# Attention scores from raw fp32 queries and keys in quarter-array tiles, values as the stationary operand, rows divided before the transposes

## The chip, the cores and the metric

The kernel runs on one core of a Trainium2 chip. The metric is the device time of the whole program in microseconds (us). The engines are PE (TensorE: matmul; PEld: its weight loads), DVE (VectorE), ACT (ScalarE), POOL (GpSimd) and SP, which here only issues transfers. Two executions of this kernel count as different from about 0.3%.

## The reference, cut to what matters

```
q, k, v: (4 batches, 8 heads, 576 positions, 64) fp32
scores = q k^T / 8
kth    = 32nd largest of each row of scores
scores = where(scores >= kth, scores, -1e9) - row maximum
attn   = exp(scores);  attn = attn / (sum(attn) + 1e-9)
x      = (attn v), heads side by side: 2304 rows x 512
h = x w_in (512x2048);  g = h / (1 + exp(-1.702 h));  x2 = g w_out (2048x512)
out = (((x2 w1) * (x2 w2)) w3) w_out2      (w1, w2: 512x1024; w3: 1024x1024; w_out2: 1024x512)
```

Row `kth` needs the scores close to full fp32 precision, since a wrong choice among near-equal scores changes the result.

## The kernel before, in words

The 2304 rows are eight chunks of 288 queries. A chunk is 18 tiles of 128 score rows: two groups of four heads, each with one "left" tile (the last 32 queries of all four heads) and eight full tiles (one head, 128 queries). One tile has 128 rows of 576 scores. The loops of all engines go by slots, one per tile; in a slot each engine does its share for several tiles at different stages: PE makes the scores of the tile two ahead, DVE searches the current and the previous one, ACT and POOL mask and exponentiate the tile two behind, and PE transposes the probabilities and weighs the values of the tile three behind. Each slot also holds one or two of the 32 units of the first feed-forward block, for the chunk before (12 fp16 matmuls a unit); units 0 to 15 give hidden rows and need a tanh, a gate product on DVE (L1014) and a split in high and low parts (ACT L865, POOL L1250); units 16 to 31 multiply by w_out. The first chunks carry other work in their place: the product of the two last weights on PE, peaks and splits of the weights on DVE. The order is written out by hand in each engine's `step`; engines meet only by counting semaphores. The search on DVE is four MAX8 and three MATCH_REPLACE8 over the 576 scores of a tile. After all chunks the second feed-forward block runs in six blocks of 384 rows, a stage of its own.

Scores (L545 to 564). Queries and keys arrive with the 64 head dimensions on partitions, twice, on both halves (L372). ACT rounds them to fp32r with a mask over the halves (`round_q`, `round_k`, L738 to 755), and POOL subtracts to get the low parts (`prepare`, L1198), so that one stationary holds high and low parts on 128 rows, and the stacked keys hold both too. A full tile is then two stationaries by two halves of the keys: four matmuls of 288 columns. A left tile needs sixteen. These preparations run nine tiles ahead, in slots 0 to 5 of each nine.

Values (L577 to 591). The transposed probabilities (L566; five transposes in a tile, copied from PSUM by ACT in two pieces, L798 and L799) are the stationary operand, the values the moving one: five fp32 matmuls of 64 columns in a full tile, 256 in a left tile. Each fp32 matmul stands as two in the records. ACT scales the result by the inverse sum (`copy_output`, L802 to 819), PE transposes it into x_T (`transpose_x`, L593), ACT takes the high part (L821) and DVE the low part (L1023). In the first chunk SP waits for the splits before it loads the next queries into the single buffer (L380).

Of the kernel before, what the change touches and what calls it, by code (L numbers as in the profile page):

```python
# [19 lines left out]
FP32 = mybir.dt.float32  # L20
# [3 lines left out]
ALU = mybir.AluOpType  # L24
# [14 lines left out]
NT = CT * NCHUNK  # L39
KB = S // P  # L40
# [78 lines left out]
class Tile:  # L119


    def __init__(self, chunk, s):
        self.chunk, self.s = chunk.next(s // CT), s % CT
        self.fixed = CT * self.chunk.off + self.s
        self.g, self.r = self.s // GT, self.s % GT
        self.left = self.r == 0
        self.h, self.j = self.g * HG + (self.r - 1) // 2, (self.r - 1) % 2
# [13 lines left out]
    def makes_xt(self):  # L141

        return self.left or self.h % 2 == 1

    def xt_count(self, extra=0):

        before = sum(Tile(Chunk(0), i).makes_xt() for i in range(self.s))
        return self.chunk.count(XT, before + extra)


XT = sum(Tile(Chunk(0), i).makes_xt() for i in range(CT))
# [52 lines left out]
def build(nc, q_in, k_in, v_in, w_in_d, w_out_d, w1_d, w2_d, w3t_d, wo2_d, out_d, x2_d, w3o_d):  # L204
# [14 lines left out]
    kst = sb("k_stack", [P, 2, HG, S], FP32R)  # L219
    kx = sb("k_stage", [P, HG, S], FP32)  # L220
    vn = sb("v_rows", [P, KB + 1, DM], FP32)
    qx = sb("q_stage", [P, HG, CHUNK], FP32)
    qs = [sb("q_high_low", [P, 2, HG, FULL], FP32R), sb("q_low_high", [P, 2, HG, FULL], FP32R)]

    DIAG = P + LEFT
    ql = [sb("q_left_high_low", [P, 2, HG * DIAG], FP32R), sb("q_left_low_high", [P, 2, HG * DIAG], FP32R)]
    attn_end = place[0]
# [5 lines left out]
    pt = sb("probs_T", [P, (KB + 1) * P], FP32)  # L233
    xn = sb("x_rows", [P, 2, 2, P], FP32)
    xl = sb("x_left", [P, 2, P], FP32)
# [17 lines left out]
    low_rows = sb("low_rows", [P, 2], FP32)  # L253
# [17 lines left out]
    at = pinned["k_stack"]  # L271
# [23 lines left out]
    ptp = nc.alloc_psum_tensor("probs_T_ps", [P, 512], FP32)  # L295
    pte = nc.alloc_psum_tensor("probs_T_end_ps", [P, 512], FP32)
    xp = nc.alloc_psum_tensor("values_ps", [P, 512], FP32)
    xtp = nc.alloc_psum_tensor("x_T_ps", [P, 512], FP32)
    mp = [nc.alloc_psum_tensor(f"ff_ps{i}", [P, 512], FP32) for i in range(2)]
    yp = [ps[:, 0, :], ps[:, 1, :], xp[:, :]]  # L300

    sem = nc.alloc_semaphore
    q_loaded, k_loaded, v_loaded = sem("q_loaded"), sem("k_loaded"), [sem("v_loaded0"), sem("v_loaded1")]
# [6 lines left out]
    q_rounded, k_rounded = sem("q_rounded"), sem("k_rounded")  # L310
    q_split, k_split = sem("q_split"), sem("k_split")
    edge_set = sem("edge_set")
    ident_set, zeros_set, rows_set = sem("ident_set"), sem("zeros_set"), sem("rows_set")
# [4 lines left out]
    transposed, pt_copied, av_done, o_copied = sem("transposed"), sem("pt_copied"), sem("av_done"), sem("o_copied")  # L318
    xt_made, xt_high, xt_low = sem("xt_made"), sem("xt_high"), sem("xt_low")
# [12 lines left out]
    def new_keys(tile):  # L332

        return tile.chunk.off % 2 == 0

    def xt_parts(t, dst):

        par = t.chunk.off % 2
        if not t.left:
            return [(slice(0, P), dst[:, par, t.h // 2, t.j * P:(t.j + 1) * P], xtp[:, 0:P])]  # L340
        parts = []
        for odd in range(2):
            rows = slice(odd * D, (odd + 1) * D)
            parts.append((rows, dst[rows, par, 2 * t.g:2 * t.g + 2, FULL:CHUNK],
                          xtp[rows, 0:P].rearrange("d (a b q) -> d b a q", a=2, b=2)[:, odd, :, :]))
        return parts
# [12 lines left out]

    def left_view(t, g):  # L360
        return t[:, g, :].rearrange("p (h c) -> p h c", c=DIAG)[:, :, 0:LEFT]

    with nc.Block() as block:

        @block.sync
        def _(sp):
# [11 lines left out]
            def load_q(chunk, g):  # L378

                wait(sp, q_split, chunk.count(20, 10 * g))  # L380
# [163 lines left out]
        def _(pe):  # L544
# [32 lines left out]
            def weigh_values(t):  # L577
                if not t.exists():
                    return
# [728 lines left out]
```

## Time and profile before

| | us |
|---|---|
| runs of the kernel | 1268.56, 1271.26, 1271.35; median 1271.26 |
| the profiled execution, its own time | 1267.95 |
| its span, first to last instruction | 1266.2 |
| PE busy (share of the span) | 1177.3 (93%) |
| DVE busy | 935.1 (74%) |
| ACT busy | 788.4 (62%) |
| POOL busy | 512.4 (40%) |

PE records overlap: a matmul is shown from its issue to its modelled end, so PE's cost in a stretch is read from the starts of successive groups and not from their durations. Shares over the whole span mix three stages (loads at the start, slots, second feed-forward block).

### The profile page before, as it was taken

The page shows a single profiled execution, that of the slowest core. Times are in us where ns is not written, and L with a number is a line of the kernel's source. Part 1 is how long each engine was busy: PE and PEld are TensorE (multiplying, and loading weights), DVE is VectorE, ACT ScalarE, POOL GpSimd, SP SyncE. Part 2 cuts the span into 40 slices and gives each one's busy share as a digit, 9 for nine tenths or more (in the row PEclk, how much of TensorE's full clock was granted, in tenths as well). Part 3 has the DMA queues.
Part 4 walks back from the last instruction along what each step waited for, and adds up shares of the span by engine and source line. Part 5 has one row for each costly group of instructions (what it writes and reads, how often), then busy time and mean ns, then how long its engine had stood idle before and what let it go on. Part 6 is the DMA issues. An engine that isn't in the chain of part 4 may idle for free.

```text
span 1266.2 us, 24613 instructions
## 1 busy us (share of the span) xinstructions
PE 1177.3 (93%) x7798; PEld 987.7 (78%) x7798; DVE 935.1 (74%) x1974; ACT 788.4 (62%) x1806; POOL 512.4 (40%) x763
## 2 busy tenths in 40 slices
PE   2699988899999999999989999999989999999999
PEld 2566566687788777878768787887768999999998
DVE  4999999999999998999899899999342311302302
ACT  3655678878977977886796887797473222222211
POOL 4533345946645665674475665554230000000000
PEclk9799997999999999999999999999999999999999
DMA  9915143311012020000202100000141011011000
GB/s 285 363 49 171 51 129 94 102 45 37 1 30 64 22 62 30 25 20 16 65 20 67 48 2 25 16 2 6 69 175 40 17 33 50 8 41 50 0 25 25
DMA packets 29866, 75.38 MB, mean 60 GB/s; under 512 B 2480, under 2 KB 14256, under 8 KB 27824
## 3 DMA queue, kind: packets, MB, share of 16 engines
q1 hardware_dynamic: 29744, 73.93, 18.7%
q8 instruction: 55, 0.90, 0.3%
q14 instruction: 67, 0.55, 0.1%
HBM read 62.39 MB, written 11.53 MB: 58 GB/s over the span
## 4 chain that ended last, share of the span: by engine, by line
PE 58%; DVE 17%; issue 12%; ACT 7%; POOL 3%; DMA 1%; POOLq 0%; ACTq 0%; SPq 0%; DVEq 0%
PE ff_ps L633 33%; PE values_ps L589 10%; PE scores_ps L633 5%; PE scores_ps L561 4%; PE values_ps L633 3%; DVE search L990 2%; PE probs_T_ps L574 2%; DVE search L996 2%; DVE top L987 2%; DVE top L979 2%; DVE peaks L1032 2%; DVE search L984 2%; ACT penalty L781 1%; ACT probs_T L798 1%; DVE gate L1014 1%
## 5 line engine op out<-in xcount | busy, mean ns | idle before, releaser
L1227 POOL TENSOR_TENSOR scores<-scores,penalty 128x576 f32<-128x576 f32 x144 | 203.5, 1413 | 209.8 <-ACT penalty L781 209.8
L589 PE MATMUL values_ps<-v_rows,probs_T 128*128 128x64 f32 (+3 forms) x1440 | 228.8, 297 | 45.8 <-ACT probs_T L799 38.4
L589 PEld LDWEIGHTS values_ps<-v_rows,probs_T 128*128 128x128 f32 (+1 forms) x1440 | 196.9, 195 | 93.1 <-ACT probs_T L799 58.7
L1160 DVE TENSOR_TENSOR ab_T<-a_sb,ff_ps 128x384 f32<-128x384 f32 x48 | 26.6, 554 | 211.1 <-PE ff_ps L633 211.1
L633 PE MATMUL ff_ps<-x_T_high,w_in_high 128*128 128x288 f16 x512 | 151.2, 295 | 2.8 <-ACT gate L856 2.8
L633 PE MATMUL ff_ps<-g_high,w_out_high 128*128 128x288 f16 x512 | 147.5, 288 | 2.4 <-DVE w_out_low L1019 1.2
L633 PE MATMUL ff_ps<-x_T_low,w_in_high 128*128 128x288 f16 x512 | 149.8, 292 | 0.0
L633 PE MATMUL ff_ps<-x_T_high,w_in_low 128*128 128x288 f16 x512 | 149.6, 292 | 0.0
L633 PE MATMUL ff_ps<-g_high,w_out_low 128*128 128x288 f16 x512 | 146.4, 286 | 0.0
L633 PE MATMUL ff_ps<-g_low,w_out_high 128*128 128x288 f16 x512 | 146.4, 286 | 0.0
L1250 POOL TENSOR_TENSOR g_low<-gate,g_high 128x288 f16<-128x288 f32 x128 | 98.9, 774 | 79.4 <-ACT g_high L865 79.4
L633 PE MATMUL ff_ps<-x_high,w_high 128*128 128x384 f32 x384 | 128.4, 334 | 0.8 <-issue 0.8
L789 ACT ACTIVATE scores<-scores,edges 128x576 f32<-128x576 f32 x144 | 111.8, 776 | 27.4 <-POOL scores L1227 27.3
L633 PE MATMUL ff_ps<-x_high,w_low 128*128 128x384 f32 x384 | 128.3, 334 | 0.0
L633 PE MATMUL ff_ps<-x_low,w_high 128*128 128x384 f32 x384 | 128.3, 334 | 0.0
L781 ACT ACTIVATE penalty<-scores,edges 128x576 f32<-128x576 f32 x144 | 111.0, 771 | 26.6 <-POOL edges L1235 25.8
L979 DVE MAX8 top<-scores 128x8 f32<-128x576 f32 x144 | 107.8, 749 | 5.7 <-ACT scores L770 3.7
L770 ACT ACTIVATE scores<-scores_ps 128x576 f32<-128x576 f32 x144 | 92.3, 641 | 26.5 <-PE scores_ps L561 26.3
L987 DVE MAX8 top<-search 128x8 f32<-128x576 f32 x144 | 107.6, 747 | 0.6
L999 DVE MAX8 top<-search 128x8 f32<-128x576 f32 x144 | 106.7, 741 | 0.0
L993 DVE MAX8 top<-search 128x8 f32<-128x576 f32 x144 | 106.6, 740 | 0.0
L990 DVE MATCH_REPLACE8 search<-top,search 128x576 f32<-128x576 f32 x144 | 106.6, 740 | 0.0
(116 smaller groups left out, 2733.1 us busy)
## 6 DMA issues: line engine op xcount, KB each, us to landing
q_stage<-q_T SPq DMA_DIRECT2D x32, 288.0 KB, 4.3
k_stage<-k_T SPq DMA_DIRECT2D x16, 576.0 KB, 8.1
x_scratch<-x_out SPq DMA_DIRECT2D x32, 144.0 KB, 1.7
x_T<-x_scratch SPq DMA_DIRECT2D x6, 768.0 KB, 4.7
out<-y_out SPq DMA_DIRECT2D x18, 256.0 KB, 2.0
v_rows<-v_rows_in SPq DMA_DIRECT2D x8, 512.0 KB, 3.5
w_T<-w_T_in SPq DMA_DIRECT2D x1, 4096.0 KB, 26.8
whole_weight<-w_in SPq DMA_DIRECT2D x2, 2048.0 KB, 10.8
```

What stands on the lines that cost most here:

```text
L589: last = nc.tensor.matmul(xp[:, 0:n], pt[0:rows, j * P:(j + 1) * P], vn[0:rows, j, first:first + n], start=j == 0, stop=j == KB)
L633: last = nc.tensor.matmul(out, stationary[i], moving[j], start=first and n == 0, stop=last_one and n == 2)
L770: act.activation(sc[:, t.ring(RING), :].rearrange("p (a b) -> p a b", a=2), ps[:, :, 0:HALF], ACT.Copy).then_inc(s_copied, 1)
L781: act.activation(pen[:, :], sc[:, t.ring(RING), :], ACT.Relu, bias=thr[:, r:r + 1], scale=-PENALTY).then_inc(pen_done, 1)
L789: act.activation(sc[:, t.ring(RING), :], sc[:, t.ring(RING), :], ACT.Exp, bias=negm[:, r:r + 1], scale=SCALE, accum_out=total[:, r:r + 1]) ...
L979: nc.vector.max(tops[:, 0:8], row).then_inc(search_a, 1)
L987: nc.vector.max(tops[:, 8:16], rest).then_inc(search_a, 1)
L990: nc.vector.match_replace(rest, tops[:, 8:16], rest, FLOOR).then_inc(search_a, 1)
L993: nc.vector.max(tops[:, 16:24], rest).then_inc(search_b, 1)
L999: nc.vector.max(tops[:, 24:32], rest).then_inc(search_b, 1)
L1227: pool.tensor_tensor(row, row, pen[:, :], ALU.subtract).then_inc(masked_done, 1)
L1250: pool.tensor_tensor(gt[1][:, u, :], gf[:, u % FF_RING, :], gt[0][:, u, :], ALU.subtract).then_inc(g_low, 1)
```

## The change

- Scores: queries and keys are used as loaded, in fp32. `scores` issues, for a full tile, four matmuls of 64 rows by 64 query columns by 288 keys, at the four 64-by-64 positions of the array: the row half picks the half of the keys (and its own PSUM bank), the column half picks 64 of the 128 queries. A left tile has eight, of 64 rows by 32 columns. Rounding, splitting and their buffers go, on ACT, POOL and (at the start) DVE. Queries and keys have a buffer for each group of heads, so their loads wait for `qk_done` of the previous user of that buffer.
- Probabilities: POOL multiplies the exponentials by the inverse sum over the whole row (`normalise`, in the slot of `invert`, between its gate work and `scale_edges`), before the transposes. The transposes and the values move one slot later (`slot.next(-4)`). The fifth transpose takes the last 128 columns in place of 64, and ACT copies 640 columns at once into one of two buffers.
- Values: the values (128 positions by 64) are stationary, the transposed probabilities move, 128 columns in a full tile, 32 in a left one. Two heads form a group: they write partitions 0 to 63 and 64 to 127 of one PSUM tile, so x arrives transposed. `copy_output` and `transpose_x` go; ten groups a chunk in place of ten x_T transposes.

```diff
+                    parts = [(i, slice(FULL, CHUNK), i * LEFT) for i in range(HG)]
                 else:
+                    first = t.j * P
+                    parts = [(t.h % HG, slice(first + c, first + c + D), c) for c in (0, D)]
+                for i, queries, col in parts:
                     for half in range(2):
+                        rows = slice(half * D, (half + 1) * D)
+                        last = nc.tensor.matmul(ps[col:col + queries.stop - queries.start, half, 0:HALF],
+                                                qx[rows, t.g, i, queries],
+                                                kx[rows, t.g, i, half * HALF:(half + 1) * HALF],
+                                                start=True, stop=True, tile_position=(half * D, col))
...
+                for pair in members:
+                    for j in range(KB + 1):
+                        for odd, (tile, head, queries, cols) in enumerate(pair):
+                            first = (t.g * HG + head) * D
+                            last = nc.tensor.matmul(
+                                out[odd * D:(odd + 1) * D, cols], vn[:, j, first:first + D],
+                                pt[:, tile.ring(2), j * P + queries.start:j * P + queries.stop],
+                                start=j == 0, stop=j == KB)
...
+            def normalise(t):
+                if not t.exists():
+                    return
+                wait_alone(pool, recip_done, t.count(1), passed_pool)
+                r = t.ring(4)
+                row = sc[:, t.ring(RING), :]
+                pool.tensor_scalar(row, row, rinv[:, r:r + 1], 1.0, ALU.mult, ALU.mult).then_inc(norm_done, 1)
...
                     subtract_penalty(slot.next(-2))
                     for c, u in second_unit(slot.next(-2)):
                         low_gate(c, u)
-                    prepare(slot)
                     for c, u in first_unit(slot.next(-1)):
                         low_gate(c, u)
+                    normalise(slot.next(-3))
                     scale_edges(slot.next(-1))
...
-                    transpose_probs(slot.next(-3))
+                    transpose_probs(slot.next(-4))
                     scores(slot.next(2))
...
-                    weigh_values(slot.next(-3))
+                    weigh_values(slot.next(-4))
...
-                    transpose_x(slot.next(-4))
```

## Rows read from the trace of the kernel before

**Rows 1.** Stretches: us; busy (count) of PE, PEld, DVE, ACT, POOL; clock; DMA

```profile
23.60:144.00 120.40, 103.47 (x446) 70.20 (x447) 118.72 (x231) 67.96 (x146) 47.18 (x73) 0.93 0.53 172
144.00:267.40 123.40, 106.94 (x670) 81.78 (x669) 123.24 (x243) 99.96 (x219) 70.48 (x94) 0.93 0.34 100
267.40:888.00 620.60, 593.21 (x4523) 495.73 (x4521) 597.38 (x1346) 503.49 (x1223) 366.63 (x547) 0.99 0.11 29
960.00:1266.00 306.00, 302.22 (x1617) 283.77 (x1614) 63.31 (x105) 70.84 (x124) 0.00 (x0) 1.00 0.08 29
```

**Rows 2.** DVE in order of time: first search step of chunks 2 and 7

```profile
267.42 0.75 DVE L979 MAX8 top<-scores 128x8 f32<-128x576 f32 x1
...
789.55 0.75 DVE L979 MAX8 top<-scores 128x8 f32<-128x576 f32 x1
```

**Rows 3.** DVE in order of time, inside one slot with gates

```profile
617.17 0.74 DVE L993 MAX8 top<-search 128x8 f32<-128x576 f32 x1
617.83 0.44 DVE L1014 SCALAR_TENSOR_TENSOR gate<-tanh,gate 128x288 f32<-128x288 f32 x1
618.18 0.08 DVE L984 MATCH_VALUE_LOAD search<-top,scores 128x8 f32 x1
...
618.92 0.08 DVE L996 MATCH_VALUE_LOAD search<-top,search 128x8 f32 x1
...
619.64 0.15 DVE L1007 RECIPROCAL inverse_total<-total_eps 128x1 f32<-128x1 f32 x1
```

**Rows 4.** The gate product L1014: its durations (min/median/max), and its group

```profile
L1014 DVE SCALAR_TENSOR_TENSOR gate<-tanh,gate x128: 430/448/1680, 183.8 to 942.5; 128x288 f32<-128x288 f32 x128
...
L1014 DVE SCALAR_TENSOR_TENSOR gate<-tanh,gate 128x288 f32<-128x288 f32 x128 | 75.7, 595 | 11.3 <-ACT gate L856 11.2
```

**Rows 5.** The chain that ended last, 487 to 498 us: start, us, work

```profile
487.63 0.44 PE probs_T_ps L574 x4
...
488.17 0.52 PE scores_ps L561 x4
488.69 1.49 PE ff_ps L633 x12
490.18 1.20 PE values_ps L589 x10
...
492.95 0.11 PE x_T_ps L604
...
495.62 2.37 PE values_ps L589 x10
```

**Rows 6.** PE in order of time: fp32 matmuls of 512 columns; a left tile's scores

```profile
101.03 1.88 PE L625 MATMUL ff_ps<-wo_sb,w_T 128*128 128x512 f32 x4
102.81 2.59 PE L589 MATMUL values_ps<-v_rows,probs_T 128*128 128x256 f32 x10
...
618.87 0.51 PE L561 MATMUL scores_ps<-k_stack,q_left_high_low 128*128 128x288 f32 x2
...
621.07 0.30 PE L633 MATMUL ff_ps<-x_T_high,w_in_high 128*128 128x288 f16 x1
```

**Rows 7.** Groups on ACT: name, shapes, count | busy us, mean ns | idle before

```profile
L817 ACT ACTIVATE x_rows<-values_ps,inverse_total 128x64 f32<-128x64 f32 x128 | 40.0, 312 | 44.2 <-PE values_ps L589 33.1 <-issue 8.5 <-DVE inverse_total L1007 2.1
...
L746 ACT ACTIVATE q_high_low<-q_stage,low_rows 128x1024 fp32r<-128x1024 f32 x16 | 18.4, 1147 | 3.7 <-DMA q_stage<-q_T 3.7
```

**Rows 8.** Groups on POOL, the same columns

```profile
L1227 POOL TENSOR_TENSOR scores<-scores,penalty 128x576 f32<-128x576 f32 x144 | 203.5, 1413 | 209.8 <-ACT penalty L781 209.8
...
L1182 POOL TENSOR_TENSOR q_low_high<-q_stage,q_low_high 128x256 fp32r<-128x256 f32 x64 | 49.2, 780 | 3.6 <-ACT q_low_high L746 3.6
...
L1266 POOL MEMSET q_left_high_low<- 128x1280 f32 x1 | 1.2, 1164 | 0.0
```

**Rows 9.** The start: first use of the keys, first matmul

```profile
11.66 1.25 ACT L754 ACTIVATE k_stack<-k_stage,low_rows 128x1152 fp32r<-128x1152 f32 x1 [4.17 <-DMA k_stage<-k_T]
...
18.70 0.82 PE L561 MATMUL scores_ps<-k_stack,q_left_high_low 128*128 128x288 f32 x2 [18.70 <-POOL q_left_low_high L1182]
```

More of the change, by code:

```diff
@@ L39 @@
 NT = CT * NCHUNK
+PADDED = (S // P + 1) * P
+GROUPS = 10
 KB = S // P
@@ L139, in ring, with ends_group, group, group_count @@
         return self.fixed % n
[L141 to L151, printed above, removed]
+    def ends_group(self):
+        return self.r % 2 == 0
+    def group(self):
+        return self.g * (GROUPS // 2) + (self.r + 1) // 2
+    def group_count(self, extra=0):
+        return self.chunk.count(GROUPS, self.group() + 1 + extra)
 def wait(eng, sem, value):
@@ L331, in build, with xt_place, xt_source @@
                                                      sem("y_copied"), [sem(f"y_stored{t}") for t in range(3)])
-    def new_keys(tile):
-        return tile.chunk.off % 2 == 0
-    def xt_parts(t, dst):
+    def xt_place(t, dst):
         par = t.chunk.off % 2
[L339 to L346, printed above, removed]
+        if t.left:
+            return dst[:, par, 2 * t.g:2 * t.g + 2, FULL:CHUNK]
+        return dst[:, par, t.h // 2, t.j * P:(t.j + 1) * P]
+    def xt_source(t):
+        out = xq[t.group() % 2]
+        if t.left:
+            return out[:, 0:2 * LEFT].rearrange("p (a q) -> p a q", a=2)
+        return out[:, 0:P]
     def piece_place(i, part):
@@ L581, in weigh_values @@
                     pe.wait_ge(v_loaded[t.g], t.chunk.batch_count(32, 32))
-                pe.wait_ge(pt_copied, t.count(1))
-                wait(pe, o_copied, t.count())
-                first, n = (t.g * HG * D, HG * D) if t.left else (t.h * D, D)
-                for j in range(KB + 1):
-                    rows = KR if j == KB else P
-                    last = nc.tensor.matmul(xp[:, 0:n], pt[0:rows, j * P:(j + 1) * P],
-                                            vn[0:rows, j, first:first + n], start=j == 0, stop=j == KB)
@@ L606, in spread_peaks @@
-            def spread_peaks(which, first, n, before):
+                wait(pe, xt_low, t.group_count(-2))
+                wait_alone(pe, pt_copied, t.count(1), passed_pe)
+                out = xq[t.group() % 2]
+                if t.left:
+                    members = [[(t, 2 * pair + odd, slice((2 * pair + odd) * LEFT, (2 * pair + odd + 1) * LEFT),
+                                 slice(pair * LEFT, (pair + 1) * LEFT)) for odd in range(2)] for pair in range(2)]
+                else:
+                    members = [[(t.next(odd - 1), t.next(odd - 1).h % HG, slice(0, P), slice(0, P))
+                                for odd in range(2)]]
```

230 lines of the change are left out of this document (57 added, 173 removed).

## The prediction

> **What bounds the kernel now.** I read the busy times by stretch first, because the page's shares mix stages. In the second feed-forward block, 960 to 1266 us, PE is busy 302 of 306 us [rows 1], and the change touches nothing there: these 306 us stay. In the slots DVE is as full as PE. From 23.6 to 144 us it is busy 118.7 of 120.4, from 144 to 267.4 us 123.2 of 123.4, and from 267.4 to 888 us 597.4 of 620.6 [rows 1]; in the last stretch PE shows 593.2, but its records overlap. The timeline of DVE gives the period: chunk 2 begins at 267.42 and chunk 7 at 789.55 [rows 2], five chunks in 522.1 us, so 104.4 us a chunk. 620.6 us are 5.94 such chunks, so DVE works 597.4 / 5.94 = 100.5 us in each and stands still for 3.9. That it really works is seen inside a slot: a MAX8 holds it 0.66 us (617.17 to 617.83), a gate 0.35, a replace with its load 0.73 (618.18, 618.92, 619.64) [rows 3], each beginning when the one before lets go.
>
> PE's load has to be summed from starts. The chain of waits shows a stretch with PE alone on it: transposes 0.54 (487.63 to 488.17), scores 0.52, a unit 1.49 (the other kind 1.58; I take 1.53), values of a full tile 1.20, of a left tile 2.37, x_T 0.11 [rows 5]; a left tile's scores take 621.07 - 618.87 = 2.20 [rows 6]. A chunk holds 32 units (49.0), 18 tiles of transposes (9.7), 16 full and 2 left scores (8.3 + 4.4 = 12.7), values (19.2 + 4.7 = 23.9) and 10 x_T (1.1): 96.4 us. So DVE (100.5) and PE (96.4) are both close to the period of 104.4; speeding up PE, ACT or POOL can win at most the 3.9 us of DVE's idleness in each of the six steady chunks, 23 us, while slowing PE by more than some 6% costs in full.
>
> **The scores on PE.** The price of an fp32 matmul is in the product of the last weights: four records of 512 columns from 101.03 to 102.81 [rows 6], 0.445 us each, 0.87 ns a column, and each matmul is two of them. 288 columns are 0.25 us a record, where the fp32r matmul of before takes 0.52 / 4 = 0.13 and is one record. A full tile after has four matmuls, so eight records. End to end they would be 2.0 us; if the four array positions work at once, 0.5. The trace of before has no matmul on part of the array, so these are the bounds. I take a case between: the two records of one matmul need the same part of the array and must follow each other; if PE starts matmuls in program order, the second record of one runs beside the first of the next, and n matmuls take n + 1 records: 5 x 0.25 = 1.25 us for a full tile, 9 x 0.25 = 2.25 for a left one. A chunk: 16 x 1.25 + 2 x 2.25 = 24.5 us, 11.8 more than before.
>
> The Trainium skill, in "TensorE: Matmul & The Clock Gate", part 3 (Packing small matmuls), has matmuls at different positions start about 4 ns apart but keep program order in start and end. Its measured cases count one record each; by its order rule the staircase holds, by its concurrency figures alone the 0.5 us would.
>
> **The values on PE.** A pair of full tiles is ten matmuls of 128 columns, 0.11 us a record: 2.2 us end to end, 1.2 as a staircase, against 2 x 1.20 + 0.11 before. With a stationary of 64 columns in place of 128 the weight load, which bounds the old records at 0.12 us, should halve; it then just fits. A left group is twenty matmuls of 32 columns, where half of 0.12 us bounds each of 40 records: 2.4 us, as now. A chunk: 8 x 1.2 + 2 x 2.4 = 14.4 us against 25.0, 10.6 less. Scores and values together: +1.2, PE 97.6 us a chunk.
>
> **The change of array shape.** Each tile's scores stand between full-array work, two changes in each of 18 slots, and each of ten groups of values has two more: 56 a chunk. The trace shows no such change. The lower bound is nothing; the nearest row for the other end is the tail of a matmul: 0.30 us for one whose successors start every 0.12 us [rows 5, 6], so 0.17 us during which nothing new could enter if the array had to be empty. A weight load, shorter than the 0.12 us at which the old value records follow each other [rows 5], can run in most of that tail, and I take 0.07: 3.9 us a chunk, PE 101.5. At 0.17 it would be 9.5, PE 107.1.
>
> **ACT and POOL.** ACT loses eight groups, the largest L817 with 40.0 us and among the others the rounding, 1.15 us in one piece in the slots that have it [rows 7]; it was never the bound, but PE and DVE waited behind these pieces. That is where part of the 3.9 us comes from, and I count on getting about half of it. POOL loses five groups of splits, the largest 49.2 us [rows 8], and gains 144 products of 576 columns with one tensor input. These are not in the trace. Below stands a memset, 1164 ns for 1280 columns, 0.52 us for 576; above, the two-input operation on 576 columns, 1.41 us [rows 8]. I take 0.9, 16 us a chunk beside some 19 of the splits removed: no change of load. Its position has a price: POOL's next operation behind it is `scale_edges`, for which ACT's mask and then POOL's subtraction wait; and the transposes now wait for it too, one slot later than before, which gives that slot back.
>
> DVE's gate has a median of 448 ns but a mean of 595 and a maximum of 1680 [rows 4], so it is held up by something for 2.3 us a chunk; the splits on POOL were running at the longest of them, and the new product will run there in every slot. I leave the sum as it is. DVE's own work falls only by the halved low part of the left tiles, 0.5 us a chunk.
>
> **The start.** The keys are used at 11.66 us, the first matmul starts at 18.70 [rows 9]. Without rounding and splits 7 us go. The first tile's matmuls cost a little more, so I take 6; the lower bound is nothing, if the loads that now start earlier push the first ones aside. Chunks 0 and 1 are DVE's (1.7 and 0.2 us of idleness [rows 1]): 1 us.
>
> **Sum.** A steady chunk after is PE's: 101.5 us and some 2.5 of waits, 104.0 against 104.4; six chunks, -2 us. With the start -6 and chunk 0 -1: -9 us on the profiled execution's own 1267.95 us (its span and 1.75 around it), 1259; that execution is 3.3 below the median of the runs, so 1262 is what I expect of a median.
>
> **Rivals.**
> - *All four positions at once.* Scores 0.5 us in every tile, 9 a chunk; PE falls to 49.0 + 9.7 + 9 + 14.4 + 3.9 = 86. DVE then sets the slots: 100 and 1 of waits, 101; six chunks -20, start and chunk 0 -7: 1244. For it: the operands lie on separate halves and banks. Against: two records per matmul in a fixed order.
> - *The array empties at each change of shape (the slower side).* 0.17 us x 56: PE 107.1, with 2.5 of waits 109.6; six chunks +31, less 7: 1295. It decides from about 0.10 us a change, where PE with its waits passes the old period by what the start gives. For it: the tail that every PE record shows. The Trainium skill speaks for this one: "TensorEngine Tiling (Array Packing)", Key Properties, says that a change of tiling mode (not of tile) drains the engine. No run so far shows it, and the page gives no time.
> - *No concurrency at all.* Scores 16 x 2.0 + 2 x 4.0 = 40, values 8 x 2.2 + 4.8 = 22.4: PE 121, with the changes 125; +21 x 6 = +126, less 6 for the start: 1391. For it: nothing of before overlaps two matmuls beyond their tails. Against: position and banks are given for each.
> - *The product on POOL in DVE's way.* If it takes 1.41 us and holds every second gate for half its length, DVE gains 8 x 0.7 = 5.6 us a chunk, 106 with waits 108: +3.6 x 6 = +22, less 7: 1286. Against: most of POOL's slot is free.
>
> **Chances.** Forecast 0.32, all four at once 0.22, emptying 0.24, no concurrency 0.11, POOL in the way 0.11. The range runs from 1236 (the first rival with fewer waits) to 1305 (emptying with a weight load exposed too) and leaves out mainly the serial case; the forecast's own range is 1250 to 1276. No change means within 0.3% (4 us), about what a measurement tells. Faster: 0.22 and three quarters of the forecast, 0.47; the same 0.10; slower 0.43.
>
> **What would show it.** The starts of the score matmuls of one full tile: 1.25 us to the next unit's first (staircase), 0.5 or 2.0. The gap from the last transpose to the first score matmul, and from the last score to the first unit: the change of shape. The group of POOL's product: 0.9 us. First matmul near 12 us. The first search steps of successive chunks: 104 us apart. DVE idle for much more than 4 us a chunk means that PE bounds; DVE with longer gates, that POOL is in the way. If the second feed-forward block is not 306 us, or chunks 0 and 1 are slower, the account is wrong in a place that I did not look at.

## The result, and the profile after

The changed kernel takes 1249.22 us (median of 4 runs, 1248.64 to 1250.4) against 1270.67 for the kernel before (4 runs): a ratio of 0.9835, 95% interval 0.9818 to 0.9852, so 21.5 us faster where 9 were forecast. The profiled execution took 1249.15 us with a span of 1246.9. The time is near the first rival's 1244 and inside the range; the forecast's own range, 1250 to 1276, is just missed. Where a run's cores show a much lower granted clock its time is left out (one run of f3 below: 1773.28 us at a granted clock of 0.57).

The stretches of the changed kernel, in the columns of [rows 1]: the first two chunks, chunks 2 to 7, and 300 us of the second feed-forward block.

```profile
18.58:144.00 125.42, 91.97 (x558) 44.84 (x554) 124.83 (x246) 56.39 (x103) 44.81 (x69) 0.99 0.56 185
144.00:267.00 123.00, 95.72 (x838) 61.29 (x838) 121.52 (x244) 86.04 (x168) 74.73 (x89) 0.93 0.34 97
259.49:869.87 610.38, 536.52 (x5179) 365.79 (x5178) 608.29 (x1335) 418.74 (x906) 351.87 (x524) 0.96 0.11 30
940.00:1240.00 300.00, 299.14 (x1608) 281.53 (x1606) 63.34 (x105) 70.22 (x123) 0.00 (x0) 1.00 0.08 28
```

The first search step of each chunk on DVE gives the account. It stands at 18.58 us against 23.60 at the start (-5.0); chunk 0 takes 117.7 us against 120.4, chunk 1 123.2 against 123.4, chunks 2 to 7 together, here and below up to the first search step of their last tile, 610.4 against 620.3 (-9.9), and what follows is 1.4 less. With -2.9 for chunks 0 and 1 that is 19.3 us of span, as the two spans say (1246.9 against 1266.2).

In chunks 2 to 7 DVE is now busy 608.3 of 610.4 us: it stands still for 2.1 us, where it stood still for 23.2. The largest of its waits in the kernel before (us in total, times, longest) was for ACT's high part of x_T, and it is gone:

```profile
DVE x_T_low L1028 <- ACT x_T_high L831: 15.3, 20, 2.0
```

DVE sets the slots. That it won only 9.9 of those 21 us is because its own work grew. The groups of its gate product and of x_T's low part, then PE's waits in chunks 2 to 7:

```profile
L949 DVE SCALAR_TENSOR_TENSOR gate<-tanh,gate 128x288 f32<-128x288 f32 x128 | 95.4, 749 | 9.5 <-ACT gate L796 9.5
L962 DVE SCALAR_TENSOR_TENSOR x_T_low<-x_T_ps,scale,x_T_high 128x128 f16<-128x128 f32 x64 | 21.0, 328 | 9.4 <-ACT x_T_high L772 9.4
```

```profile
PE probs_T_ps L567 <- POOL scores L1139: 69.4, 54, 3.4
PE x_T_ps L591 <- ACT probs_T L761: 0.7, 2, 0.4
```

The mean gate of the whole run is 749 ns against 595 [rows 4]. PE waits 69 us for POOL's product, and this costs nothing that shows, since PE has the time (e2). PE in order of time, a full tile's scores between transposes and a unit, a pair of values, and a left tile's scores and values:

```profile
463.56 0.71 PE L567 MATMUL probs_T_ps<-identity,scores 128*128 128x128 f32 x5
464.19 0.72 PE L553 MATMUL scores_ps<-keys,queries 64*64 64x288 f32 x8
464.84 0.30 PE L622 MATMUL ff_ps<-g_high,w_out_high 128*128 128x288 f16 x1
...
470.85 1.31 PE L591 MATMUL x_T_ps<-probs_T,v_rows 128*64 128x128 f32 x20
472.10 0.30 PE L622 MATMUL ff_ps<-g_high,w_out_high 128*128 128x288 f16 x1
...
486.01 1.36 PE L591 MATMUL x_T_ps<-probs_T,v_rows 128*64 128x32 f32 x40
487.30 0.30 PE L622 MATMUL ff_ps<-g_high,w_out_high 128*128 128x288 f16 x1
...
499.99 0.71 PE L553 MATMUL scores_ps<-keys,queries 64*32 64x288 f32 x16
500.63 0.30 PE L622 MATMUL ff_ps<-x_T_high,w_in_high 128*128 128x288 f16 x1
```

From start to next start: transposes 0.63, scores 0.65 in a full tile and 0.64 in a left one, values 1.25 and 1.29. A chunk is 49.0 (units) + 18 x 0.65 + 18 x 0.65 + 8 x 1.25 + 2 x 1.29 = 85.0 us of PE, against 96.4 before. The answer to the gate of [rows 3] is DVE and then POOL in order of time around 501 us:

```profile
501.12 0.74 DVE L928 MAX8 top<-search 128x8 f32<-128x576 f32 x1
501.78 1.22 DVE L949 SCALAR_TENSOR_TENSOR gate<-tanh,gate 128x288 f32<-128x288 f32 x1
502.93 0.08 DVE L919 MATCH_VALUE_LOAD search<-top,scores 128x8 f32 x1
```

```profile
498.49 0.75 POOL L1139 TENSOR_SCALAR scores<-scores,inverse_total 128x576 f32<-128x576 f32 x1
...
501.28 1.41 POOL L1114 TENSOR_TENSOR scores<-scores,penalty 128x576 f32<-128x576 f32 x1 [1.13 <-ACT penalty L743]
502.65 0.94 POOL L1145 TENSOR_TENSOR g_low<-gate,g_high 128x288 f16<-128x288 f32 x1
```

The gate begins half a us after POOL's subtraction of the penalty and ends 0.31 us after it, at 502.69 + 0.31. I went through all 96 gates of chunks 2 to 7. Of the changed kernel 54 begin beside that subtraction, and all of them end 0.31 to 0.33 us behind it; together they take 35.0 us more than 0.44 each. Another 38 begin with nothing running on POOL, which starts its next small operation 0.16 to 0.27 us into them: they average 0.43. The last four begin beside the product (0.58 on average). All 96 are 35.2 over; this sum is called their excess below. Before, 9 lay beside the subtraction (4.4 us over), 9 beside a split of the keys (6.1), 25 beside the low part of a gate (4.5), 15.2 in all. So 20.0 us were given back here. The search step at 501.12 lies beside the same operation and keeps its 0.74.

In the slot of [rows 3] the kernel before starts the same subtraction only after the gate, which began at 617.83:

```profile
618.42 1.43 POOL L1227 TENSOR_TENSOR scores<-scores,penalty 128x576 f32<-128x576 f32 x1 [0.84 <-ACT penalty L781]
```

Over chunks 2 to 7 it stood all over the slot there, at 3.4 us after the slot's first search step in the median; in the changed kernel nine in ten subtractions begin 0.5 to 0.8 us after that step (median 0.62), and the gates behind the search at 1.33.

### The profile page after: what moved, and what is told of

Read it like the earlier page. It is cut to its first block, busy times and chain, and to the rows that moved or that the text cites. A ratio compares the mean times of both kernels' runs of the same rounds, so it can differ in the third digit from the quotient of the medians.

```text
span 1246.9 us, 25714 instructions
## 1 busy us (share of the span) xinstructions
PE 1090.3 (87%) x8710; PEld 803.0 (64%) x8710; DVE 939.3 (75%) x1954; ACT 668.4 (54%) x1374; POOL 488.6 (39%) x714
## 4 chain that ended last, share of the span: by engine, by line
DVE 39%; PE 28%; issue 27%; DVEq 2%; ACT 1%; DMA 1%; POOL 0%; SPq 0%; POOLq 0%; ACTq 0%
PE ff_ps L622 20%; DVE search L925 8%; PE scores_ps L622 5%; DVE search L919 5%; DVE top L922 5%; DVE search L931 5%; DVE top L914 4%; DVE gate L949 3%; PE x_T_ps L622 3%; DVE peaks L966 2%; DVEq L160 2%; DVE top L934 1%; DVE top L928 1%; DVE inverse_total L942 1%; DMA v_first_quarter<-v_rows_in 1%
## 5 line engine op out<-in xcount | busy, mean ns | idle before, releaser
L567 PE MATMUL probs_T_ps<-identity,scores 128*128 128x128 f32 x720 | 113.6, 291 | 117.6 <-POOL scores L1139 115.1
L567 PEld LDWEIGHTS probs_T_ps<-identity,scores 128*128 128x128 f32 x720 | 82.8, 146 | 157.4 <-POOL scores L1139 151.4
L1139 POOL TENSOR_SCALAR scores<-scores,inverse_total 128x576 f32<-128x576 f32 x144 | 121.1, 841 | 100.6 <-DVE inverse_total L942 100.6
L622 PE MATMUL ff_ps<-x_T_high,w_in_high 128*128 128x288 f16 x512 | 154.9, 303 | 2.9 <-ACT gate L796 2.9
L622 PE MATMUL ff_ps<-x_T_low,w_in_high 128*128 128x288 f16 x512 | 154.0, 301 | 0.0
L1145 POOL TENSOR_TENSOR g_low<-gate,g_high 128x288 f16<-128x288 f32 x128 | 103.5, 809 | 87.4 <-ACT g_high L805 87.4
L553 PE MATMUL scores_ps<-keys,queries 64*64 64x288 f32 (+1 forms) x1280 | 114.7, 466 | 21.4 <-DMA keys<-k_T 11.6
L591 PE MATMUL x_T_ps<-probs_T,v_rows 128*64 128x128 f32 (+1 forms) x1920 | 108.8, 264 | 9.2 <-ACT probs_T L761 7.7
L591 PEld LDWEIGHTS x_T_ps<-probs_T,v_rows 128*64 128x64 f32 x1920 | 92.0, 142 | 35.5 <-issue 35.5
L922 DVE MAX8 top<-search 128x8 f32<-128x576 f32 x144 | 107.0, 743 | 0.0
## 6 DMA issues: line engine op xcount, KB each, us to landing
keys<-k_T SPq DMA_DIRECT2D x16, 576.0 KB, 8.1
whole_weight<-w_in SPq DMA_DIRECT2D x2, 2048.0 KB, 15.2
```

The lines of the kernel that those rows point to most:

```text
L553: last = nc.tensor.matmul(ps[col:col + queries.stop - queries.start, half, 0:HALF], qx[rows, t.g, i, queries], kx[rows, t.g, i, half * HAL ...
L567: last = nc.tensor.transpose(ptp[:, j * P:(j + 1) * P], row[:, min(j * P, S - P):min((j + 1) * P, S)], ident[:, :])
L591: last = nc.tensor.matmul(out[odd * D:(odd + 1) * D, cols], vn[:, j, first:first + D], pt[:, tile.ring(2), j * P + queries.start:j * P + q ...
L622: last = nc.tensor.matmul(out, stationary[i], moving[j], start=first and n == 0, stop=last_one and n == 2)
L922: nc.vector.max(tops[:, 8:16], rest).then_inc(search_a, 1)
L1139: pool.tensor_scalar(row, row, rinv[:, r:r + 1], 1.0, ALU.mult, ALU.mult).then_inc(norm_done, 1)
```

## The experiments

Chunks are the distances of first search steps. Every time is a median of 3 or more runs, and every ratio is to runs of the kernel before that were taken with them (medians 1268.3 to 1270.7 us), so small differences between sets of runs are safer in the ratios. Chunks and gates are of the one profiled run of each kernel. "Gate first" is the first edit below; most later kernels have it, and are compared with the kernel that has it too.

**e1, gate first.** The first gate product is issued ahead of the first two search steps, before POOL's subtraction begins.

```diff
+                    for c, u in first_unit(old):
+                        gate(c, u)
                     search(new, 0)
                     search(old, 4)
-                    for c, u in first_unit(old):
-                        gate(c, u)
```

> The changed kernel with one move on DVE: the first gate product of a slot stands before the two search steps that open the slot, not behind them. Nothing else. Theory A (DVE sets the slots; its first gate is held while POOL subtracts the penalty, which in the changed kernel begins 0.6 to 1.0 us after the slot's first search step, just ahead of the gate at 1.3 us): the gates fall back from 0.75 us mean to about 0.46, and since DVE is on the path the time falls by most of the 39 us that all gates now last beyond 0.44 us: 1249 to about 1218 (1210 to 1228). Theory B (the new product on POOL holds the gates): it lies 3 to 5 us into the slot and the move changes nothing for it: 1249 within 4 us. Theory C (PE and its wait for the product set the slots): within 4 us, whatever the gates do.

1219.15 us (1217.08 to 1221.95), ratio 0.9621 [0.9599, 0.9643]: 30 us less than the changed kernel (27 by the ratios). Chunks 2 to 7 take 582.7 us, and the excess of their gates is 7.1 us. That is 27.7 us less in the steady chunks, all but exactly the 28.1 that the gates lost. The group, and the same place in a slot, DVE and POOL:

```profile
L949 DVE SCALAR_TENSOR_TENSOR gate<-tanh,gate 128x288 f32<-128x288 f32 x128 | 63.2, 497 | 13.3 <-ACT gate L796 10.8 <-issue 1.9
```

```profile
492.42 0.44 DVE L949 SCALAR_TENSOR_TENSOR gate<-tanh,gate 128x288 f32<-128x288 f32 x1
492.79 0.75 DVE L914 MAX8 top<-scores 128x8 f32<-128x576 f32 x1
```

```profile
490.72 0.74 POOL L1139 TENSOR_SCALAR scores<-scores,inverse_total 128x576 f32<-128x576 f32 x1
...
492.99 1.41 POOL L1114 TENSOR_TENSOR scores<-scores,penalty 128x576 f32<-128x576 f32 x1 [0.88 <-ACT penalty L743]
```

The subtraction now begins when the gate has ended. Of the 7.1 us of excess that are left, 5.6 lie beside the product.

**e2, the product narrow.** POOL multiplies 32 of 576 columns (the rest of the rows is left undivided, with the scale of the values lowered to match).

```diff
-                row = sc[:, t.ring(RING), :]
+                row = sc[:, t.ring(RING), 0:32]
```

> The changed kernel with POOL's division product over the first 32 of the 576 columns only (the other columns are left undivided, and the values' scale is 64 times lower so that all numbers stay finite): it leaves out most of the division. The product falls from 0.84 us to about 0.25. Theory A (the subtraction holds the first gates): gates still last 0.75 us in the mean, the time stays at 1249 within 5 us. Theory B (the product holds the gates): gates 0.5 us, time down by 15 to 30 us. Theory C (PE waits for the product, and that wait is on the path): 0.6 us less in each slot's chain, time down by 20 us or more with the gates as they are.

1247.61 us, ratio 0.984 [0.9818, 0.9861]: 1.6 us less, within what a measurement tells. Gates 735 ns. POOL's product is not what the changed kernel pays for.

**e3 and e6, scores twice**, without and with the gate first: each tile's score matmuls are issued twice.

```diff
-                for i, queries, col in parts:
+                for i, queries, col in parts + parts:
```

> The changed kernel with every score matmul issued twice (the second set overwrites the first with the same numbers). From the traces a tile's scores take 0.65 us, of which 0.5 are the matmuls: +0.5 us in each of 144 slots, 72 us of PE work, PE from about 85 us a chunk to 94. Theory A (DVE sets the slots at 102.5 us a chunk): at most +8 us. Theory C (PE sets them): +40 to +72. If the eight records of a tile don't overlap as the starts suggest, a tile's block grows by more than 0.6 us.

> The kernel with the gate first, with every score matmul issued twice: +0.48 us a slot on PE as the same edit showed on the changed kernel, PE from 85 to about 94 us a chunk, close to the 96 of the kernel before, beside a DVE of 97. Theory E (PE's load so near to DVE's is what made DVE wait before): +2 to +3.5 us a chunk, 1231 to 1241. Theory D (ACT's pieces did): within 5 us of 1219.

e3: 1246.44 us (1238.79 to 1253.87), ratio 0.9848 [0.9798, 0.9898], so 0.48 us more in each of 18 tiles (a full tile's block is 1.13 us), 8.6 us of PE a chunk, cost nothing that can be told: in chunks 2 to 4 of the profiled run 0.1 to 0.5 us each. That run, the fastest of four that lie 15 us apart, even won some us from chunk 5 on (101.5 and 97.4 in chunks 5 and 6 against 104.4 and 102.0), where the subtraction fell off the gate: 30 gates beside it in place of 54, excess 22.6 us. e6, where no such thing is to be won: 1228.92, ratio 0.9686 [0.9662, 0.9711], 9.8 us over e1 and between the two theories. DVE waits 9.2 us for ACT's copy ahead of the gate. PE's load is cheap, not free, once DVE is relieved.

**e4, one row half.** The full tiles as two matmuls of 64 rows by 128 columns, both on the lower row half (so the second half of the keys is read from the lower copy). **e9, two row halves**: the same two matmuls, one on each row half; on e1, with the change of `parts` alone.

```diff
-                    parts = [(t.h % HG, slice(first + c, first + c + D), c) for c in (0, D)]
+                    parts = [(t.h % HG, slice(first, first + P), 0)]
...
-                        rows = slice(half * D, (half + 1) * D)
+                        rows = slice(half * D, (half + 1) * D) if t.left else slice(0, D)
...
-                                                start=True, stop=True, tile_position=(half * D, col))
+                                                start=True, stop=True, tile_position=(half * D if t.left else 0, col))
```

> The changed kernel with the full tiles' scores as two matmuls of 64 rows by 128 columns, both on the lower 64 rows of the array (the queries and keys lie there too), so that neither position half nor row half can work beside the other; left tiles as they are. Four records of 288 columns. If a record costs 0.24 us as in full-array work and the four positions had really worked at once, the block from the first score matmul to the next unit grows from 0.65 us to about 1.1; if the positions don't overlap and a record on part of the array is only cheaper, it stays at 0.65 or falls. Time: theory A (DVE sets the slots), +0.5 us of PE in 128 slots is absorbed, at most +8 us; theory C, +40 to +60.

> The changed kernel with the first gate product ahead of the search (1219.2 us), its full score tiles as two matmuls of 64 rows by 128 columns, one on each row half, in place of four of 64 by 64. Theory H (the row halves run beside each other, two records of 0.25 us each in turn): the block stays at 0.62 to 0.68 us and the time at 1217 to 1222 us; the column halves bring nothing. Theory I (only four small tiles run beside each other, and 64 by 128 tiles go one after the other): 4 records in series, a block near 1.15 us, as the tiles on one row half alone took, PE 8 us a chunk longer, and 1222 to 1230 us.

A tile's scores and the next unit, first of e4 and then of e9:

```profile
472.58 1.23 PE L553 MATMUL scores_ps<-keys,queries 64*128 64x288 f32 x4
473.75 0.30 PE L622 MATMUL ff_ps<-g_high,w_out_high 128*128 128x288 f16 x1
```

```profile
471.49 0.76 PE L553 MATMUL scores_ps<-keys,queries 64*128 64x288 f32 x4
472.17 0.30 PE L622 MATMUL ff_ps<-g_high,w_out_high 128*128 128x288 f16 x1
```

Four records on one row half take 1.17 us: they start 0.24 apart (the second 0.35 behind the first), and the unit starts 0.34 behind the last. The same four on two row halves take 0.68, and eight on four positions 0.65; there the first four records start within 0.02 us of each other and the other four 0.29 later. So positions run fully beside each other, two records of one after another each; e9 takes 1218.81 us (ratio 0.9598 [0.9581, 0.9616]), the same as e1. The two row halves alone do it; splitting the queries over the column halves brings nothing. e4's time is a miss: 1235.73 us (1226.98 to 1238.83), ratio 0.9721 [0.968, 0.9763], 13.5 us *faster* than the changed kernel with 8 us a chunk more of PE. Only 27 gates lie beside the subtraction (13.8 us), which begins 1.5 us into the slot in the median, where the changed kernel has 0.62. A slower PE moved the phase and freed most gates: excess is 18 us less, idleness of DVE 5 more.

**e5 and f3, the load put back**, on e1 and on idle scratch: e5 ACT's scaled copies and roundings, f3 POOL's subtractions (256, 128 and 576 columns) in the slots that had them. **e14** has both. The core of f3:

```diff
+                pieces = [(0, 256)] + ([(256, 256)] if t.r <= 3 else []) + ([(512, 128)] if t.r in (1, 5) else [])
+                if t.r >= 2 and t.chunk.off % 2 == 0 and not (t.chunk.reg is None and t.chunk.off == 0 and t.g == 0):
+                    pieces.append((640, 576))
+                for first, n in pieces:
+                    last = pool.tensor_tensor(spare[:, 2, first:first + n], ...
```

> The kernel with the gate first (1219 us), with ACT's removed load put back as idle copies: in the slots where the kernel before rounds, copies of 1024 and 128 or of 1152 columns between spare buffers, and a copy of 64 columns in every slot, at the place where they stood. It computes the same. Question: DVE stood still 3.9 us a chunk before the change and 0.4 after it; what freed it? Theory D (ACT's pieces were in the way): 2 to 3.5 us of DVE idleness a chunk come back, 1219 to 1231 to 1241. Theory E (PE's load was, at 96 us a chunk beside DVE's 97 to 100): within 5 us of 1219.

> The changed kernel with the first gate product ahead of the search steps (1219.2 us), with subtractions of the old widths (256, 256, 128 and 576 columns, on idle scratch) put back on POOL in the slots where the kernel before had them; every result is the reference's. Theory D: +15 to +24 us, so 1234 to 1243 us, and DVE's gates and search steps longer where POOL's subtractions lie beside them. Theory E (POOL's splits cost DVE nothing): 1218 to 1222 us, as ACT's rounding put back gave 1220.6.

> The changed kernel with the first gate product ahead of the search, and both loads put back on idle scratch: ACT's scaled copies and roundings and POOL's subtractions. Theory M (the preparation works through POOL's and DVE's meeting; ACT adds little): 1249 to 1254 us, against 1249.1 with POOL's alone. Theory N (the two add up in the queue that passes between ACT and POOL): 1256 to 1268 us, as much as the kernel before with the same order of gates (1266.2), so that PE's lighter load and the start would be worth nothing once the preparation is there.

e5: 1220.64 us, ratio 0.9631 [0.9607, 0.9655], +1.5. f3: 1249.05 (three runs), ratio 0.9839 [0.9819, 0.9859], **+29.9** (28 by the ratios). e14: 1252.03, ratio 0.9871 [0.9834, 0.9908], +32.9. POOL's splits are what matters, more than the 15 to 24 us expected. In f3, chunks 2 to 7 take 608.2 us, 25.5 over e1, and chunk 1 5.8 more. DVE's waits in that stretch, its gate there, and POOL's subtractions:

```profile
DVE gate L952 <- ACT gate L799: 13.9, 14, 2.5
```

```profile
L952 DVE SCALAR_TENSOR_TENSOR gate<-tanh,gate 128x288 f32<-128x288 f32 x96 | 58.3, 607 | 15.8 <-ACT gate L799 13.9 <-issue 1.9
...
L1121 POOL TENSOR_TENSOR spare<-spare 128x256 f32<-128x256 f32 (+2 forms) x188 | 149.8, 822 | 0.4
```

Of the 25.5, 8.9 are longer gates (16.0 us of excess against 7.1), 1.4 the rest of DVE's work, 15.2 idleness, mostly for ACT's copy of the gate. Why that copy comes late (POOL's queue stands between ACT's operations in every slot) is not shown. The load of f3 and e14 is put beside a product on POOL that the kernel before did not have, so the two figures need not be what the preparation cost there.

**e7, e8, f1, f2, f4: the kernel before**, in all but e7 with preparation taken away from chunk 2 on (8 columns wide in place of full; the rest of queries and keys is left out; the small pieces of the left tiles stay). e7 only has the gate first; e8 also ACT's and POOL's preparation narrow, f1 only ACT's, f2 only POOL's; f4 is e8 in the old order of gates.

```diff
-                act.activation(qs[which][:, g, :, :], qx[:, :, 0:FULL], ACT.Copy, scale=mask).then_inc(q_rounded, 1)
+                cols = FULL if full_width(chunk) else 8
+                act.activation(qs[which][:, g, 0:heads, 0:cols], qx[:, 0:heads, 0:cols], ACT.Copy, scale=mask).then_inc(q_rounded, 1)
...
-                low(qs[which][:, t.g, i, :], qx[:, i, 0:FULL], q_split)
+                low(qs[which][:, t.g, i, 0:cols], qx[:, i, 0:cols], q_split)
```

> The kernel before with the same single move of the first gate product. Theory A (the move is worth what the first gates lose to POOL's port, and in the kernel before they lose 10.9 us in the six steady chunks and some more in chunk 1): 1269 to about 1257 (1253 to 1263). If the move were a gain by itself, whatever the port does, it would be worth 30 us here too: 1239. If PE's load holds this kernel, it is worth nothing.

> The kernel before with the gate first, and from chunk 2 on with the rounding on ACT and the splits on POOL over 8 columns a head in place of 256 or 576: later chunks work with partly stale queries and keys, the instructions are the same in number and order. Against the run with the gate first alone it shows what the removed preparation is worth without any change on PE. Theory D (ACT's and POOL's pieces held DVE up): -2 to -3.5 us in each of six chunks, 12 to 20 us under it. Theory E (PE's load did): within 5 us of it.

> The kernel before with the first gate product ahead of the search steps (1266.2 us, median of its runs), and from chunk 2 on ACT's masked roundings of the queries and keys only 8 columns wide; the rest of queries and keys in the buffers is left as it was, so those scores are not the reference's. POOL's splits stay full. With both narrow the kernel took 1242.6 us. Theory D (what DVE gains is bought by POOL: its 576-, 256- and 128-column subtractions hold DVE's operations or delay its own subtraction of the penalty): 1260 to 1266 us, since POOL keeps its work. Theory E (ACT's pieces of 1.15 us stand in front of exponentials and tanhs that DVE and POOL wait for): 1243 to 1249 us.

> The same kernel, with ACT's roundings full and POOL's splits 8 columns wide from chunk 2 on (the low parts of queries and keys are left out there). Theory D: 1243 to 1249 us. Theory E: 1260 to 1266 us. If each of the two gives about half of the 23.6 us, neither engine alone was what held DVE, and both theories fall in their pure form.

> The kernel before in its own order of the gates, with ACT's roundings and POOL's splits both 8 columns wide from chunk 2 on (the rest of queries and keys is left out). Theory A (relief brings POOL's subtraction of the penalty forward, into the first gate product at 1.3 us of the slot, so part of the gain is given back): 1252 to 1262 us, with first gates over 0.8 us in chunks 2 to 7, against 1242.6 us with the gate moved ahead. Theory G (the collision belongs to the changed kernel's own slot, to its product on POOL and its later transposes, and relief alone does not bring it): 1240 to 1247 us, first gates near 0.5 us.

| | us | ratio to before | chunks 2 to 7 | gates' excess |
|---|---|---|---|---|
| e7 | 1266.16 | 0.9981 [0.9964, 0.9997] | 620.1 | 16.0 |
| e8 | 1242.57 | 0.9797 [0.9773, 0.9822] | 601.0 | 4.4 |
| f1 | 1256.1 | 0.9896 [0.9878, 0.9914] | 612.7 | 13.3 |
| f2 | 1256.96 | 0.9909 [0.9891, 0.9927] | 612.8 | 5.9 |
| f4 | 1251.44 | 0.9857 [0.984, 0.9873] | 603.6 | 10.3 |

e7 is a miss: some 12 us were expected and 2 came. In the kernel before the gate meets the splits wherever it stands (19 beside them, 9.2 us, 28 beside the gate's low part, 6.7), so its place is worth nothing there. e8: without the preparation 23.6 us less. f1 and f2 fall between the two theories: each half is worth about 10 us there, and neither alone gives what both give. f4 against e8 is 8.9 us and inside neither theory. Only 2.6 of them lie in chunks 2 to 7, the others stand before, where the preparation is still full. In chunks 2 to 7 the old order has 14 gates beside the subtraction (6.4 us) where e8 has none, but the kernel before had 9 (4.4 us): relief of ACT and POOL alone brings little of the collision about. The place of the subtraction says the same: its median is 3.4 us into the slot before, 2.2 in f4, 0.62 in the changed kernel and also in e2, 0.9 in e3, 1.5 in e4. The relief of ACT and POOL moves it part of the way; with more work on PE (e3, e4) it drifts later again, so PE's relief has a share. No run has PE's relief alone.

**e10, e11, e12, e13: from here on.** On e1: the division on ACT (e10), the peak of the first quarter of the values read after the first search steps and not ahead of them (e11), both (e12), and the later peak with the division on POOL in the first 36 slots and on ACT after (e13).

```diff
+                act.activation(row, row, ACT.Copy, scale=rinv[:, r:r + 1]).then_inc(norm_done, 1)
...
-            see_v(0)
...
+            return slot.chunk.reg is not None or slot.fixed >= 2 * CT
```

> The changed kernel with the first gate product ahead of the search, the rows divided by ACT in place of POOL. Theory A (DVE sets the slots, POOL's product lies where no gate product is): no gain, and ACT is asked for some 0.6 to 0.75 us more in each slot, 100 us in all, in front of its exponentials and tanhs: 1219 to 1232 us. Theory J (POOL's product holds DVE back by 2 us or more a chunk): 1195 to 1212 us.

> The changed kernel with the first gate product ahead of the search, and the peak of the first quarter of the values read in slot 0 behind the search, not ahead of all of it. Theory K (the first search waits for that load at 16.0 us and its 2.55 us of reduction, while the first scores are there some us earlier): the first search begins 2 to 5 us earlier, the 2.5 us come back inside chunk 0, and the total is 1215 to 1219 us. Theory L (the start is bound by the keys' and queries' loads and chunk 0 by its own loads): 1218 to 1221 us.

> Both edits together: the sum of the two differences within 2 us, if they lie at different places (the start and the slots). By theories A and K 1216 to 1230 us, by J and K 1192 to 1210 us.

> The first gate product ahead of the search, the first peak later, and the rows divided by POOL in the first 36 slots and by ACT in all later ones. With ACT dividing throughout, chunk 1 took 124.9 us against 118.4 with POOL dividing, and chunks 2 to 7 6.7 us less together. If these two differences belong to the chunks they stand in (ACT has the weights to split in chunk 1), the time is 1217.9 less 5 to 8: 1209 to 1214 us. If the loss in chunk 1 is only moved on, 1216 to 1220 us.

e10: 1221.03 us, ratio 0.9613 [0.9596, 0.963]. Chunks 2 to 7 take 576.0 us, 6.7 less than e1, with 1.3 us of gates' excess; chunk 1 takes 128.8 against 119.0: ACT splits the weights there, and DVE waits 10.1 us for it. e11: 1217.94, ratio 0.96 [0.9583, 0.9616]; the first search begins at 13.63 us, 4.8 earlier, and chunk 0 gives 3.0 of it back. e12: 1219.89, ratio 0.9617 [0.96, 0.9634], the sum. **e13: 1210.72 us** (1209.84 to 1212.22), ratio 0.9543 [0.9507, 0.9578], in the middle of what was expected and the fastest of all: 38.5 us under the changed kernel (37 by the ratios). Its steady stretch and its gate:

```profile
253.62:830.26 576.64, 519.28 (x5180) 359.88 (x5179) 574.59 (x1334) 490.63 (x1013) 265.64 (x417) 0.99 0.12 32
```

```profile
L965 DVE SCALAR_TENSOR_TENSOR gate<-tanh,gate 128x288 f32<-128x288 f32 x128 | 58.3, 458 | 12.7 <-ACT gate L808 10.6 <-issue 2.1
```

## Why the prediction was wrong

Faster was right and the range held, but the mechanism was that of the rival "all four positions at once", and the gain was more than twice the forecast's. The rival's own sum did not come true either: it had -20 us for the six steady chunks, they gave -9.9, and that its total lies near is in part luck.

1. **The step that failed: the scores as a staircase.** "The second record of one runs beside the first of the next, and n matmuls take n + 1 records", 1.25 us for a full tile and 2.25 for a left one. They take 0.65 and 0.64: 11.7 us a chunk, array changes included, where 24.5 and a share of 3.9 for the changes stood. e4 and e9 show what holds in its place: records on one position follow each other at 0.24 us, positions do not wait for each other at all. The Trainium skill's concurrency figures ("TensorE: Matmul & The Clock Gate", part 3), which I weighed and put second, were the ones that hold here. In the trace the first records of the four positions start 6 or 7 ns apart.
2. **Values.** A pair was 1.2 us in the sum and is 1.25. A left group was 2.4 by half of an old weight load for each record; 40 records take 1.29, 0.03 each, so half of the old price is no bound here. 14.4 a chunk became 12.6.
3. **The change of shape.** 0.07 us each, 3.9 a chunk in the sum. The starts of the changed kernel give it: transposes take 0.64 us ahead of scores and 0.55 ahead of a unit, a unit 1.57 ahead of values and 1.48 elsewhere; behind the last score record the unit starts after 0.34 where score records follow at 0.24, behind the last of a pair of values after 0.20 where they follow at 0.11. That is 0.09 us at each change, 5.2 us for 56, so this term was too small. It is not the rival's 0.17, and with the scores at 0.65 us it could not decide: the rival of 1295 falls, and so does serial execution.
4. **The bound.** This followed from step 1. With PE at 101.5 us the sum made PE the engine of the steady chunk and left -2 us there. With PE at 85.0 DVE sets the slots, and all but 2.1 of its 23.2 idle us went. e3 shows it: 8.6 us more of PE a chunk cost less than can be told.
5. **ACT and POOL.** "I count on getting about half" of DVE's idleness, and "no change of load" for POOL. The split load was worth far more than that: 23.6 us in the kernel before (e8 against e7), 32.9 put back on e1 (e14). With both back the kernel stands 14.1 us under e7. That is what PE's relief, the start and the rest are worth beside the preparation, of which the start is 5. The sum had looked for the loads' cost in busy time alone; it was in collisions and in waits passed on.
6. **The product on POOL.** 0.9 us in the sum, 0.84 measured on average and 0.75 in the steady slots. The rival in which it holds every second gate falls by e2. What the rival had right is that POOL would hold DVE's gate: but with its subtraction of the penalty, an old operation that came earlier in the slot (0.62 us in place of 3.4). I left "2.3 us a chunk" of held gates in the sum as it was; it became 5.9 (35.2 / 6). Most of the gain that did not arrive was lost here, as e1 shows by getting 28 us of it back.
7. **Start and early chunks.** -5.0 for the start against -6, for another reason than the sum's: PE has its first scores at 11.6 us, but DVE first waits until 16.1 for a quarter of the values, and reads its peak for 2.5 us (e11). Chunks 0 and 1 gave -2.9 against -1. The second feed-forward block is unchanged, as said.

In sum: -19.3 of span is -5.0, -2.9, -9.9 and -1.4; the steady term of -9.9 is -21.1 of idleness, +20.0 of gates and -8.8 of DVE's other work (x_T's low part 22.8 to 18.8 us, the rest spread over all its steps and without a cause shown).

Why the gate is held and the search steps are not, the runs show only as a pattern: the gate reads two tensors, search steps one. The Trainium skill has the rule ("SBUF — State Buffer", "SBUF: two separate sides" and "Who interferes with whom"): DVE's second port pair is GpSimd's only one, an exclusive lock for a whole instruction, which a DVE operation with two SBUF inputs needs against a GpSimd operation that reads SBUF; whoever starts first keeps it. All 54 cases agree, and so do the gates that began first and kept their 0.44. It shows from the other side too: three gates of e1 and eight of f2 begin less than 0.1 us behind an operation of POOL and keep 0.43 to 0.45 us, and that operation takes 1.05 to 1.09 us in place of 0.75. That rule of the Trainium skill, laid over the timeline of the slot, would have given the cost of a gate beside POOL ahead of any run; the prediction left it out. That the subtraction would move ahead of the gate it does not say. Open is the way by which POOL's splits make ACT's copy late in f3.

## What to carry to other kernels

When a change relieves several engines at once, price the phase and not only the load: list, for the engine that will then be the bound, which of its operations are held by a neighbour's, and ask where that neighbour's operation will stand once its own wait is gone. Then try the order of issue on the bounding engine first; here one moved instruction was worth 27 to 30 us, more than the whole change, and it was worth 2 in the kernel before. A heavier engine that makes a kernel faster (e4) is a sign that a phase, not a load, is being measured.

## What the runs showed of the hardware

- Small fp32 score matmuls of 288 columns at different positions of the array overlap fully: 8 records at four positions 0.65 us, 4 at two positions 0.68, 4 at one position 1.17, 16 at four positions 1.13 (e6: 472.97 to 474.10). The 16 records of a left tile, 32 columns of the array wide, take 0.64 as well.
- Between full-array matmuls and matmuls on part of the array each change, in or out, took 0.09 us on PE (changed kernel: transposes 0.64 against 0.55 us, units 1.57 against 1.48, last score record to unit 0.34 against 0.24).
- DVE's scalar_tensor_tensor with both inputs in SBUF (0.44 us) that begins beside a running POOL operation of 0.7 to 1.4 us ends 0.31 to 0.33 us after it, in all 54 cases of the changed kernel, up to 1.52 us long; one that began first is not held. MAX8 and MATCH_REPLACE8 beside the same operation keep 0.73 to 0.75 us. Their means differ more between sets of runs than by POOL's load: 733 ns in e13 and 737 with both loads back in e14 of one set, 748 in f1 and f2 and 754 with the load back in f3 of another.
- POOL's multiplication of 128x576 fp32 by a column of scalars takes 0.75 us alone, ACT's 0.78, POOL's subtraction of two such tensors 1.41.
